# First attention half of a three-block kernel: state updates after even groups, outputs after odd ones, gate rows spread over more groups, products of queries and keys first

## The chip, the cores and the metric

The kernel runs on one core of one Trainium2 chip, in float32 (many matmul operands are split into two fp32r parts, "hi" and "lo", whose products are added). The metric is the device time of one execution in microseconds. The core has TensorE (PE) for matrix products, VectorE (DVE), ScalarE (ACT) and GpSimd (POOL) for element-wise work, and SyncE (SP), which here only issues DMA transfers. Each engine works through its own list of instructions in program order; they meet through semaphores that one engine increments and another waits for.

## The reference, cut to what matters

```
# attention: 2 batches, 8 heads, 768 tokens, head size 40
for t in range(S):
    m_new = maximum(f_gate[t] + m, i_gate[t])
    f_stab = exp(f_gate[t] + m - m_new); i_stab = exp(i_gate[t] - m_new)
    C = f_stab * C + i_stab * outer(v[t], k[t])
    n = f_stab * n + i_stab * k[t]
    h = C @ q[t];  denom = maximum(abs(n . q[t]), 1)
    y[t] = sigmoid(o_gate[t]) * h / denom
# first block: mixes tokens, then channels (x is y of all heads, 768 x 320 per batch)
h = relu(xT @ w_tok1) @ w_tok2;  u = x + hT
x = u + relu(u @ w_ch1) @ w_ch2
# second block: a 2-D Fourier transform, a layer norm, two channel layers
u = x + real(fft2(x));  un = (u - mean) / sqrt(var + 1e-6)
out = u + relu(un @ w_ch1') @ w_ch2'
```

## The kernel before

The recurrence over 768 tokens is worked out in chunks of 128 tokens: 6 chunks per batch, `cc` = 0 to 11 (`NCC`), the first six being batch 0. A chunk has two groups of 4 heads, so there are 24 groups `n` (`NG`); `cc = n // 2`, `g = n % 2`. The change lies in groups 0 to 11, batch 0 ("the first half").

For one group, in the order of the data:

- `log_weights(n)` on TensorE (lines 438 and 442): a mask and the product of two small matrices `L` and `R`, which hold the gates' logarithms, into one PSUM bank.
- `attend(n)` on ScalarE: the exponential of that bank is `W` (line 831). There is one such bank, so `log_weights(n + 1)` waits until `W` of group n is out of it.
- `products(n)` on TensorE (line 456): keys times queries, into one of two banks, so it waits until `scores(n - 2)` has read that bank.
- `scores(n)` on VectorE (line 1112): `S`, product times weight. `S` and `W` have two buffers each.
- `in_chunk(n)` on TensorE (line 480): `S` times the values, into the output bank of the chunk. `from_state(cc)` (line 465) adds what the state gives, `to_state(cc)` (line 489) makes the state's increment, `decays(cc)` (line 518) the decay factors.
- `update_state(cc)` on VectorE (lines 1103, 1105) adds the increment to `C`, after `to_state(cc)`. `finish(cc)` on VectorE (lines 1076 to 1087, five instructions) divides and gates the output: the finished rows of `xt`.
- `result_hi(cc)` on ScalarE (line 823) and `result_lo(cc)` on GpSimd (line 1390) split these rows into `x_hi` and `x_lo`, which `mix_tokens` on TensorE (line 533) reads.

The gates are prepared in three parts of 256 tokens by `gate_rows(part, step)` on VectorE, steps 0 to 8 (lines 1013 to 1046); part 2 is spread over groups by the table `GATE_AT`, which gives for a group n the steps that follow its scores. `spread_rows(cc)` (line 1062) makes `R` for a chunk, `spread(cc)` on ScalarE (line 797, for the second half also line 800) makes `L`. ScalarE and GpSimd also split the weights of the later layers piece by piece (lines 772 and 1397, table `SPLIT_AT`). At group 7 ScalarE has three more copies of 8 x 768 (lines 853 to 855).

TensorE begins with `WARM_UP` = 7 matmuls on constant data (line 627). Its loop over n of the first half is: `log_weights(n + 2)`, `products(n + 2)`, for odd n `from_state`, then `in_chunk(n)`, for even n `decays`, for odd n `to_state` and (from n = 5 on) `mix_tokens(0, (n - 5) / 2)`. From group 12 on, the order is written out between layers of the first block, and the PSUM bank of the log weights gets its mask by a copy on ScalarE (line 835) that `log_weights` waits for.

VectorE's loop over n of the first half is: `scores(n)`; `rest(n)`, which for even n is `update_state(cc - 1)` and `finish(cc - 1)` and for odd n nothing; the gate rows of `GATE_AT`; for odd n below 9 `spread_rows((n + 3) // 2)`.

SyncE issues the loads of a chunk in order: keys and queries, scaled queries, values and keys (`load_kv`, waits for `to_state` of two chunks before), the output gate `og` (line 348), then pieces of weights. `gate(cc)` on ScalarE (line 808) waits for `og`.

Of the kernel before, what the change touches and what calls it, by code (L numbers as in the profile page):

```python
# [19 lines left out]
NC = S // CH  # L20
# [21 lines left out]
LN_STEPS = 2 * 6 + 1  # L42
FOLD_STEPS = 18
NEG = -1.0e30
WARM_UP = 7
FCH = [F1 // P] * NBLK + [F2 // P] * NBLK
FBASE = [sum(FCH[:k]) for k in range(2 * NBLK)]
GATE_PARTS = [(0, 2 * CH), (2 * CH, 4 * CH), (4 * CH, S)]
PART_OF = [0, 0, 1, 1, 2, 2]

SP_PIECES = {2: (2,), 3: (3,), 4: (4, 5), 5: (6, 7, 8), 6: (9, 10), 7: (11, 12), 8: (13, 14)}
GATE_AT = {1: (0,), 2: (1, 2), 3: (3, 4), 4: (5, 6), 5: (7, 8)}
SPLIT_AT = {2: (0,), 3: (1,), 4: (2,), 5: (3,), 6: (4,), 7: (5,), 8: (6,), 9: (7,), 10: (8,), 11: (9,), 13: (10,),
            14: (11, 12, 13), 15: (14,), 16: (15,), 17: (16, 17), 18: (18,)}
SPLIT_L1 = {1: 14, 2: 15, 4: 16, 6: 17, 7: 18}
# [38 lines left out]
def build(nc, a, out):  # L94
# [220 lines left out]
    with block:  # L315
# [111 lines left out]
        def _(pe):  # L427
# [199 lines left out]
                pe.matmul(BANK[n], W[0][:, 0], W[0][:, :, :].rearrange("p a b -> p (a b)"),  # L627
                          start=True, stop=True).then_inc(warm_done, 1)
            pe.wait_ge(const_ready, 2)
            for n in range(2):  # L630
                log_weights(n)
                products(n)
            for n in range(NG // 2):
                c, g = n // 2, n % 2
                if 1 <= n <= NG // 2 - 2:
# [115 lines left out]
        def _(act):  # L751
# [73 lines left out]
            def attend(n):  # L825
                cc, g = n // 2, n % 2
                act.wait_ge(logw_done, n + 1)
                if n >= 2:
                    act.wait_ge(s_done, n - 1)
                    act.wait_ge(kw_done, kw_count(n - 2))  # L830
                act.activation(W[n % 2][:, :, :].rearrange("p a b -> p (a b)"), D_BANK,
                               ACT.Exp).then_inc(w_done, 1)
                if NG // 2 - 1 <= n < NG - 1:
                    act.wait_ge(w_done, n + 1)
                    act.activation(D_BANK.rearrange("p (a b) -> p a b", b=P),
                                   f32(mask[:, :]).unsqueeze(1).to_broadcast([P, 4, P]),
                                   ACT.Copy).then_inc(mask_done, 1)
                if g == 0 and 1 <= cc < NC:
                    decay(cc)
                if n == 0:  # L840
                    select()
                if n == 0:
                    gate(0)
                if n == 1:
                    gates_hi(1)
                if n == 2:
                    sources_hi(1)
                if n == 5:
                    gates_hi(2)
                if n == 6:  # L850
                    sources_hi(2)
                if n == 7:
                    act.activation(g_ah[32:32 + H, :], g_A[32:32 + H, :], ACT.Copy).then_inc(ah_done, 1)
                    act.activation(AB[1][0:H, :], g_A[32:32 + H, :], ACT.Copy).then_inc(ab_hi, 1)
                    act.activation(AB[1][64:64 + H, :], f32(g_bh[32:32 + H, :]), ACT.Copy).then_inc(ab_hi, 1)
                if n == 9:
                    act.activation(g_ea[32:32 + H, :], g_A[32:32 + H, :], ACT.Exp).then_inc(ea_ready, 1)
                if g == 0 and cc >= 1:
                    gate(cc)
                    if cc + 1 < NCC:  # L860
                        spread(cc + 1)
                if g == 0 and 2 <= cc <= NC:
                    result_hi(cc - 2)
                if g == 1 and cc >= NC:
                    result_hi(cc - 1)
                for m in SPLIT_AT.get(n, ()):
                    if m < N_CH2:
                        split_hi(m)
# [125 lines left out]
        def _(dve):  # L994
# [120 lines left out]
            def rest(n, parts=range(2)):  # L1115

                cc, c, g = n // 2, n // 2 % NC, n % 2
                for part in parts:
                    if g == 0 and part == 0 and c >= 1:
                        update_state(cc - 1)  # L1120
                    if g == 0 and part == 1 and cc >= 1:
                        finish(cc - 1)
# [49 lines left out]
            for n in range(NG // 2):  # L1172
                scores(n)
                if n == 0:
                    for step in range(4, 9):
                        gate_rows(1, step)
                rest(n)
                for step in GATE_AT.get(n, ()):
                    gate_rows(2, step)
                if n % 2 == 1 and n < 9:  # L1180
                    spread_rows((n + 3) // 2)
                if n == 7:
                    dve.wait_ge(ab_zero, 2)
                    dve.tensor_tensor(AB[1][96:96 + H, :], g_i[32:32 + H, :], f32(g_bh[32:32 + H, :]),
                                      ALU.subtract).then_inc(gate_step, 1)
                if n == 9:
                    dve.wait_ge(ah_done, len(GATE_PARTS) + 1)
                    dve.tensor_tensor(AB[1][32:32 + H, :], g_A[32:32 + H, :], f32(g_ah[32:32 + H, :]),
                                      ALU.subtract).then_inc(gate_step, 1)
# [168 lines left out]
        def _(pool):  # L1358
# [40 lines left out]
            def attend(n):  # L1399
                cc, c, g = n // 2, n // 2 % NC, n % 2  # L1400
# [14 lines left out]
                    scale_state(cc)  # L1415
                if g == 1 and cc >= NC and c < NC - 1:
                    scale_q(cc + 1)
                if g == 0 and 2 <= cc <= NC:
                    result_lo(cc - 2)
                if g == 1 and cc >= NC:  # L1420
                    result_lo(cc - 1)
# [83 lines left out]
```

## Time and profile before

| | us |
|---|---|
| runs of the kernel before | 402.97, 394.94, 400.56; median 400.56 |
| the profiled execution, its own time | 398.74 |
| its span, first to last instruction | 397.0 |
| TensorE busy in it | 387.6 (98%) |
| VectorE, ScalarE, GpSimd busy | 191.3, 151.6, 109.2 |
| mean granted TensorE clock | 0.986 |

A timeline row reads: start in us, duration in us, engine, line, operation, output <- input, sizes, xcount, and in brackets how long the engine sat idle before it and what ended the idle time. A float32 matmul appears as two records. A matmul's record reaches past the moment at which the next can start, because matmuls are pipelined. The granted clock is 1.00 for 2.4 GHz and 0.50 for 1.2 GHz.

### The profile page before, as it was taken

What the parts mean: (1) busy time and instruction counts of PE and PEld (TensorE: products, weight loads), DVE (VectorE), ACT (ScalarE), POOL (GpSimd) and SP (SyncE); (2) the same over time, 40 slices, a digit from 0 to 9 for tenths busy, and PEclk for the clock granted to TensorE, in tenths of its full rate; (3) what the DMA queues carried; (4) which work ended last, traced back from release to release, by engine and by line L of the source; (5) the groups of instructions that cost most, each with busy time, mean ns of one, the idle gap of its engine ahead of it and who ended that gap; (6) DMA issues with size and microseconds to landing.
All of it is one profiled execution on the core that took longest, in us unless ns stands there. A gap on an engine that the chain in (4) does not pass through costs nothing.

```text
span 397.0 us, 6364 instructions
## 1 busy us (share of the span) xinstructions
PE 387.6 (98%) x2482; PEld 371.2 (94%) x2482; DVE 191.3 (48%) x396; ACT 151.6 (38%) x312; POOL 109.2 (28%) x106
## 2 busy tenths in 40 slices
PE   8998989999999999999999999999999999999997
PEld 3888978999999999999999899999999989999996
DVE  7875655654443342147912555458924373340320
ACT  5656588577462131012631034505423201240310
POOL 5355596566332000000390000623550000000000
PEclk9995999999999999999999999999999999999999
DMA  6663688433130000032121000623130000000001
GB/s 170 194 184 119 209 293 259 163 97 106 35 101 17 18 0 0 18 117 99 23 95 35 0 2 0 217 78 120 10 142 0 2 1 35 17 2 35 17 7 44
DMA packets 18277, 30.54 MB, mean 77 GB/s; under 512 B 2504, under 2 KB 10824, under 8 KB 18248
## 3 DMA queue, kind: packets, MB, share of 16 engines
q1 hardware_dynamic: 17672, 29.87, 23.8%
q8 instruction: 20, 0.33, 0.4%
q10 hardware_dynamic: 576, 0.27, 0.2%
q14 instruction: 9, 0.07, 0.1%
HBM read 26.17 MB, written 3.96 MB: 76 GB/s over the span
## 4 chain that ended last, share of the span: by engine, by line
PE 93%; ACT 2%; issue 1%; POOL 1%; DVE 1%; DMA 1%; SPq 0%; ACTq 0%; DVEq 0%; POOLq 0%
PE ps L618 28%; PE ps L597 23%; PE ps L456 5%; PE ps L724 5%; PE ps L480 5%; PE ps L600 4%; PE ps L599 4%; PE ps L704 4%; PE ps L555 3%; PE ps L533 3%; PE ps L627 2%; PE ps L465 2%; PE ps L573 2%; PE ps L489 2%; PE ps L442 1%
## 5 line engine op out<-in xcount | busy, mean ns | idle before, releaser
L903 ACT ACTIVATE h_hi<-ps 128x384 fp32r<-128x384 f32 x88 | 43.3, 492 | 118.8 <-PE ps L600 118.8
L1153 DVE SCALAR_TENSOR_TENSOR h_lo<-ps,h_hi 128x384 fp32r<-128x384 f32 x88 | 48.7, 555 | 57.2 <-ACT h_hi L903 56.8
L1159 DVE TENSOR_TENSOR xt<-ps,xt 128x320 f32<-128x320 f32 x24 | 11.8, 491 | 72.0 <-PE ps L618 71.9
L618 PE MATMUL ps<-ch_hi,h_hi 128*128 128x320 f32 x144 | 45.5, 316 | 0.0
L618 PE MATMUL ps<-ch_hi,h_lo 128*128 128x320 f32 x144 | 44.5, 309 | 0.0
L618 PE MATMUL ps<-ch_lo,h_hi 128*128 128x320 f32 x144 | 44.5, 309 | 0.0
L618 PE MATMUL ps<-m_hi,h_hi 128*128 128x320 f32 x120 | 37.5, 313 | 0.6 <-POOL m_lo L1397 0.6
L618 PE MATMUL ps<-m_hi,h_lo 128*128 128x320 f32 x120 | 37.1, 309 | 0.0
L618 PE MATMUL ps<-m_lo,h_hi 128*128 128x320 f32 x120 | 37.1, 309 | 0.0
L1397 POOL TENSOR_TENSOR m_lo<-m_raw,m_hi 128x640 fp32r<-128x640 f32 x11 | 18.1, 1668 | 56.2 <-ACT m_hi L772 56.2
L597 PE MATMUL ps<-uT_hi,ch_hi 128*128 128x384 f32 x96 | 33.0, 344 | 0.0
L597 PE MATMUL ps<-uT_hi,ch_lo 128*128 128x384 f32 x96 | 32.1, 335 | 0.0
L597 PE MATMUL ps<-uT_lo,ch_hi 128*128 128x384 f32 x96 | 32.1, 334 | 0.0
L1112 DVE TENSOR_TENSOR S<-ps,W 128x512 f32<-128x512 f32 x24 | 16.5, 685 | 25.9 <-PE ps L456 17.4
L456 PE MATMUL ps<-qz,kT 128*128 128x256 f32 x96 | 27.5, 411 | 1.4 <-DVE S L1112 1.4
L480 PEld LDWEIGHTS ps<-vs,S 128*128 128x128 f32 x192 | 25.4, 199 | 2.0 <-issue 1.3
L618 PEld LDWEIGHTS ps<-ch_lo,h_hi 128*128 128x128 f32 x144 | 27.1, 188 | 0.1
L618 PEld LDWEIGHTS ps<-ch_hi,h_hi 128*128 128x128 f32 x144 | 27.1, 188 | 0.1
L618 PEld LDWEIGHTS ps<-ch_hi,h_lo 128*128 128x128 f32 x144 | 27.0, 188 | 0.0
L597 PE MATMUL ps<-uT_lo,m_hi 128*128 128x384 f32 x80 | 26.8, 335 | 0.0
L597 PE MATMUL ps<-uT_hi,m_lo 128*128 128x384 f32 x80 | 26.8, 335 | 0.0
L597 PE MATMUL ps<-uT_hi,m_hi 128*128 128x384 f32 x80 | 26.8, 335 | 0.0
(157 smaller groups left out, 924.0 us busy)
## 6 DMA issues: line engine op xcount, KB each, us to landing
ch_raw<-in_ch SPq DMA_DIRECT2D x11, 384.0 KB, 5.4
m_raw<-in_m SPq DMA_DIRECT2D x11, 320.0 KB, 4.5
vs<-in_vs SPq DMA_DIRECT2D x12, 168.0 KB, 2.7
kT<-in_kT SPq DMA_DIRECT2D x24, 80.0 KB
qz<-in_qT SPq DMA_DIRECT2D x24, 80.0 KB
ks<-in_ks SPq DMA_DIRECT2D x12, 160.0 KB, 3.3
og<-in_o SPq DMA_DIRECT2D x12, 160.0 KB, 3.4
x_scratch<-xt SPq DMA_DIRECT2D x12, 160.0 KB, 1.8
```

The costliest lines, as they stand in the source:

```text
L456: mm = pe.matmul(p_bank(n)[:, j * 2 * CH:(j + 1) * 2 * CH], kT[:, t, 2 * g + j], qz[:, t, :, 2 * g + j], start=True, stop=True)
L480: mm = pe.matmul(y_bank(cc)[:, head * DV:(head + 1) * DV], Sx[n % 2][:, j], vs[:, cc % 2, head], start=(head == 0), stop=True, skip_group_ ...
L597: pe.matmul(bank, w[wx][:, f, dc * P:(dc + 1) * P], ux[:, dc], start=(i == 0), stop=False)
L599: pe.matmul(bank, w[0][:, f, 2 * P:3 * P], uT_x[:, :], start=False, stop=False)
L600: pe.matmul(bank, w[1][:, f, 2 * P:3 * P], uT_x[:, :], start=False, stop=True).then_inc(l1_done, 1)
L618: mm = pe.matmul(bank, h[hx][:, f, i * P:(i + 1) * P], w[wx][:, f], start=(f == 0 and hx == 0 and wx == 0), stop=(f == FCH[k] - 1 and hx = ...
L704: mm = pe.matmul(bank[0:rows_, dst:dst + n], eo[yx][:, y, start:start + rows_], seq[wx][:, first:first + n], start=(i == 0), stop=(i == le ...
L724: mm = pe.matmul(R_BANK[n % 4][:, 0:DM], UT[ux][0:rows_, m, jp * P:(jp + 1) * P], chan[wx][0:rows_, m], start=(m == 0 and ux == 0 and wx = ...
L903: act.activation(h[0][:, f], h_bank(k, f), ACT.Relu).then_inc(hhi_done, 1)
L1112: dve.tensor_tensor(Sx[n % 2][:, :, :].rearrange("p a b -> p (a b)"), p_bank(n), W[n % 2][:, :, :].rearrange("p a b -> p (a b)"), ALU.mult ...
L1153: dve.scalar_tensor_tensor(out=h[1][:, f], in0=h_bank(k, f), scalar=0.0, in1=f32(h[0][:, f]), op0=ALU.max, op1=ALU.subtract).then_inc(hlo_ ...
L1397: pool.tensor_tensor(lo, raw, f32(hi), ALU.subtract).then_inc(wlo_done, 1)
```

## The change

Four edits in the first half. The warm-up has 5 matmuls instead of 7, and after it TensorE does the products of groups 0 and 1 and then both log weights, instead of alternating. VectorE does `update_state` after the scores of an even group and `finish` after those of the odd group that follows. The gate rows of part 2 and the `spread_rows` are distributed anew (`GATE_AT`, `SPREAD_AT`; `spread_rows(2)` moves from after group 1 to after group 0). The splits of finished rows (`result_hi`, `result_lo`) of chunks 0 to 3 move one group later on ScalarE and GpSimd.

```
--- before.py
+++ after.py
@@ -42,14 +42,15 @@
-WARM_UP = 7
+WARM_UP = 5
...
-GATE_AT = {1: (0,), 2: (1, 2), 3: (3, 4), 4: (5, 6), 5: (7, 8)}
+GATE_AT = {1: (0,), 2: (1, 2), 3: (3,), 4: (4, 5, 6), 5: (7, 8)}
+SPREAD_AT = {3: 3, 5: 4, 7: 5}
...
@@ -627,9 +628,10 @@
             pe.wait_ge(const_ready, 2)
-            for n in range(2):
-                log_weights(n)
-                products(n)
+            products(0)
+            products(1)
+            log_weights(0)
+            log_weights(1)
...
@@ -859,7 +861,7 @@
-                if g == 0 and 2 <= cc <= NC:
+                if (g == 1 and 2 <= cc < NC) or (g == 0 and cc == NC):
                     result_hi(cc - 2)
...
@@ -1174,11 +1176,15 @@
                 if n == 0:
                     for step in range(4, 9):
                         gate_rows(1, step)
-                rest(n)
+                    spread_rows(2)
+                if n % 2 == 0 and n > 0:
+                    update_state(n // 2 - 1)
                 for step in GATE_AT.get(n, ()):
                     gate_rows(2, step)
-                if n % 2 == 1 and n < 9:
-                    spread_rows((n + 3) // 2)
+                if n % 2 == 1 and n > 1:
+                    finish(n // 2 - 1)
+                if n in SPREAD_AT:
+                    spread_rows(SPREAD_AT[n])
...
@@ -1415,7 +1421,7 @@
-                if g == 0 and 2 <= cc <= NC:
+                if (g == 1 and 2 <= cc < NC) or (g == 0 and cc == NC):
                     result_lo(cc - 2)
```

First place, TensorE at the start of the program. Before (`W_94` is the constant tile of the warm-up, `S_96` the scores of group 0):

```order
L627 MATMUL ps<-W_94 128x512 x7
L438 MATMUL ps<-mask,identr 128x512
L442 MATMUL ps<-R,L 128x512
L456 MATMUL ps<-qz,kT 128x256 x2
L438 MATMUL ps<-mask,identr 128x512
L442 MATMUL ps<-R,L 128x512
L456 MATMUL ps<-qz,kT 128x256 x2
L480 MATMUL ps<-vs,S_96 128x42 x4
```

The same place in the changed kernel, where line numbers are higher by one:

```order
L628 MATMUL ps<-W_94 128x512 x5
L457 MATMUL ps<-qz,kT 128x256 x4
L439 MATMUL ps<-mask,identr 128x512
L443 MATMUL ps<-R,L 128x512
L439 MATMUL ps<-mask,identr 128x512
L443 MATMUL ps<-R,L 128x512
L481 MATMUL ps<-vs,S_96 128x42 x4
```

The two warm-up matmuls are gone, and nothing stands between the two log weights now.

Second place, VectorE from the state update after group 4 to the scores of group 5 (`S_97` is the scores' buffer of odd groups; the five rows to `xt` are `finish(1)`, the two to `g_bh` are gate steps 5 and 6). Before:

```order
L1105 TENSOR_TENSOR C<-ps,C 40x4x42 x2
L1076 TENSOR_SCALAR den<-ps 128x8
L1078 SCALAR_TENSOR_TENSOR den<-ps,den 128x8
L1081 RECIPROCAL rden<-den 128x8
L1083 TENSOR_TENSOR ps<-ps,rden 128x8x40
L1087 SCALAR_TENSOR_TENSOR xt<-xe_101,ps 128x320
L1034 TENSOR_TENSOR g_fi<-g_fi,g_A 40x256
L1037 CAST g_bh<-g_fi 40x256
L1112 TENSOR_TENSOR S_97<-ps,W_95 128x512
```

The changed kernel, from the same state update:

```order
L1107 TENSOR_TENSOR C<-ps,C 40x4x42 x2
L1033 TENSOR_TENSOR g_fi<-g_fi,g_m 40x256
L1036 TENSOR_TENSOR g_fi<-g_fi,g_A 40x256
L1039 CAST g_bh<-g_fi 40x256
L1114 TENSOR_TENSOR S_97<-ps,W_95 128x512
L1044 TENSOR_TENSOR AB_102<-g_fi,g_bh 8x256
L1048 TENSOR_TENSOR AB_102<-g_A,AB_102 8x256
L1078 TENSOR_SCALAR den<-ps 128x8
L1080 SCALAR_TENSOR_TENSOR den<-ps,den 128x8
```

Five rows moved from ahead of the scores to behind them, and one gate row (step 4) came in ahead.

Third place, GpSimd in groups 4 to 6 (`kw` are weighted keys, `C` the scaling of the state that waits for `from_state(2)`, `tok_lo` a piece of weights). Before:

```order
L1408 TENSOR_TENSOR kw_91<-ks,W_94 128x4x40
L1379 TENSOR_TENSOR qs<-qs,eAb 104x512
L1390 TENSOR_TENSOR x_lo<-xt,x_hi 128x320
L1397 TENSOR_TENSOR tok_lo<-tok_raw,tok_hi 128x384
L1408 TENSOR_TENSOR kw_91<-ks,W_95 128x4x40
L1385 TENSOR_TENSOR C<-C,eAb 104x336
L1397 TENSOR_TENSOR tok_lo<-tok_raw,tok_hi 128x384
L1408 TENSOR_TENSOR kw_92<-ks,W_94 128x4x40
```

The changed kernel:

```order
L1414 TENSOR_TENSOR kw_91<-ks,W_94 128x4x40
L1385 TENSOR_TENSOR qs<-qs,eAb 104x512
L1403 TENSOR_TENSOR tok_lo<-tok_raw,tok_hi 128x384
L1414 TENSOR_TENSOR kw_91<-ks,W_95 128x4x40
L1391 TENSOR_TENSOR C<-C,eAb 104x336
L1396 TENSOR_TENSOR x_lo<-xt,x_hi 128x320
L1403 TENSOR_TENSOR tok_lo<-tok_raw,tok_hi 128x384
L1414 TENSOR_TENSOR kw_92<-ks,W_94 128x4x40
```

The `x_lo` split now stands behind the scaling of the state, which itself waits for TensorE's `from_state` of group 5.

## Rows read from the trace of the kernel before

**Rows 1.** The page: its head and the granted clock in 40 slices

```profile
span 397.0 us, 6364 instructions
...
PEclk9995999999999999999999999999999999999999
```

**Rows 2.** Waits of TensorE over the whole run: us in total, times, longest

```profile
PE ps L442 <- ACT ps L835: 1.6, 1, 1.6
...
PE ps L456 <- DVE S L1112: 1.4, 1, 1.4
...
PE ps L438 <- ACT W L831: 0.5, 1, 0.5
```

**Rows 3.** Stages: length, busy time (count) by engine, granted clock, DMA share, GB/s

```profile
31.00:32.00 1.00, 0.99 (x2) 0.83 (x3) 0.94 (x3) 0.86 (x3) 0.00 (x0) 0.53 0.69 251
...
41.00:42.00 1.00, 1.00 (x10) 0.97 (x8) 0.97 (x2) 0.00 (x0) 0.00 (x0) 0.85 0.88 302
```

**Rows 4.** Timeline of VectorE: an early cast; state update of group 4 to scores 5

```profile
6.94 0.29 DVE L1037 CAST g_bh<-g_fi 40x256 fp32r<-40x256 f32 x1
...
26.46 0.69 DVE L1105 TENSOR_TENSOR C<-ps,C 40x168 f32<-40x168 f32 x2 [1.59 <-PE ps L489]
...
28.43 0.49 DVE L1087 SCALAR_TENSOR_TENSOR xt<-xe,ps 128x320 f32<-128x320 f32 x1
...
29.38 0.97 DVE L1037 CAST g_bh<-g_fi 40x256 fp32r<-40x256 f32 x1
30.28 0.67 DVE L1112 TENSOR_TENSOR S<-ps,W 128x512 f32<-128x512 f32 x1
```

**Rows 5.** Timeline of TensorE: products 7, log weights 9, products 9, mixing, log weights 11

```profile
31.01 2.07 PE L456 MATMUL ps<-qz,kT 128*128 128x256 f32 x4 [1.39 <-DVE S L1112]
...
42.53 0.40 PE L438 MATMUL ps<-mask,identr 128*128 128x512 f32 x1
...
42.99 1.02 PE L456 MATMUL ps<-qz,kT 128*128 128x256 f32 x4
...
46.30 0.39 PE L533 MATMUL ps<-x_hi,tok_hi 128*128 128x320 f32 x1
...
49.51 0.40 PE L438 MATMUL ps<-mask,identr 128*128 128x512 f32 x1
```

**Rows 6.** The start: chain piece of products 0; timeline of VectorE; products 3

```profile
11.01 0.86 PE ps L456 x4
...
12.15 0.66 DVE L1112 TENSOR_TENSOR S<-ps,W 128x512 f32<-128x512 f32 x1
...
15.12 0.69 DVE L1112 TENSOR_TENSOR S<-ps,W 128x512 f32<-128x512 f32 x1
...
16.39 0.66 DVE L1062 TENSOR_TENSOR R<-AB,roles 40x512 fp32r<-40x512 f32 x1
...
16.27 1.02 PE L456 MATMUL ps<-qz,kT 128*128 128x256 f32 x4
```

**Rows 7.** Timeline: GpSimd's state scaling of group 7, its x_lo 4; mixing that reads it

```profile
44.96 0.76 POOL L1385 TENSOR_TENSOR C<-C,eAb 104x336 f32<-104x336 f32 x1 [4.61 <-PE ps L465]
...
60.74 0.86 POOL L1390 TENSOR_TENSOR x_lo<-xt,x_hi 128x320 fp32r<-128x320 f32 x1 [1.06 <-ACT x_hi L823]
...
61.90 0.50 PE L533 MATMUL ps<-x_hi,tok_hi 128*128 128x320 f32 x1
```

**Rows 8.** Timeline of ScalarE in groups 6 and 7; below it pieces of the chain

```profile
30.83 0.47 ACT L808 ACTIVATE xe<-og 128x320 f32<-128x320 f32 x1
...
32.94 0.58 ACT L831 ACTIVATE W<-ps 128x512 f32<-128x512 f32 x1
33.54 0.84 ACT L853 ACTIVATE g_ah<-g_A 8x768 fp32r<-8x768 f32 x1
...
53.17 0.36 ACT x_hi L823
...
55.52 0.47 PE ps L442
```

## The prediction

> **What bounds the kernel now.** I read the page first: a span of 397.0 us, and a granted clock that is full in every slice but one [rows 1]. TensorE is busy 98% of the span, so only its idle time and its slow time can be won. The waits of TensorE come next: three matter in the first 60 us, 1.4 us of products for VectorE's scores, 0.5 us for ScalarE's weights `W`, 1.6 us for ScalarE's mask copy [rows 2]. The table of stages places the slow slice: the granted clock is 0.53 in the microsecond from 31 and back at 0.85 in the one from 41 [rows 3]. So for 10 us TensorE ran at 1.2 GHz, the lower of its two levels, after having been at 2.4 GHz. What it did just before is the 1.39 us wait of products 7, which began only at 31.01 [rows 5]. The wait and the slow stretch are one event: this is where the change acts.
>
> The cause of the wait is VectorE's queue. It got the state increment at 26.46, and had to do the update (to 27.15), `finish(1)` (to 28.92) and two gate rows before the scores of group 5, which ran from 30.28 to 30.95 [rows 4]. Products 7 needs these scores because it reuses their bank. TensorE had been free for it since 31.01 - 1.39 = 29.62.
>
> **The change, part by part.** All positions are in the time scale of the trace of before.
>
> *The start.* Two warm-up matmuls go. Each streams as many columns as one pair of products, 0.86 us in the chain [rows 6]; two products move into their place, so the first log weights come about when they did. TensorE now idles between log weights 0 and 1 for one exponential, and `in_chunk(0)` waits for scores 0, which VectorE cannot begin before 12.15: end 12.81, against a start of about 13.1 before. That gives 0.3 us. Against it, `spread_rows(2)` (0.66 us) now stands before scores 1, which then end at 15.81 + 0.66 = 16.5 instead of 15.8, and products 3, which started at 16.27, waits for them 0.2 us [rows 6]. What ends the 0.5 us wait for `W` a little later is ScalarE's chain behind the decays, which starts 0.3 us sooner. With the two splits gone from group 4 and `finish(0)` gone from ahead of scores 3 (a stall under 0.2 us), I take -0.4 us up to group 5; the bounds are 0 (ScalarE is held by the DMA of `og` anyway) and -0.9 (the whole 0.5 us of the wait and 0.4 besides).
>
> *The wait and the slow clock.* In group 4 VectorE now does update, gate steps 4, 5 and 6, then scores 5. `finish` took 28.92 - 27.15 = 1.77 us, and about 0.4 us for step 4 come in, so the scores end near 30.95 - 1.77 + 0.4 = 29.6, and sooner by what the cast loses less. The cast took 0.97 us here and 0.29 us in the first part of the gates [rows 4], so the scores end between 28.9 and 29.6: just before TensorE wants them at 29.62 (both move with the start). Sum: -1.4 us.
> Of that cast the Trainium skill says more (SBUF — State Buffer, Who interferes with whom): such a cast and a GpSimd instruction exclude each other for a whole instruction. By this rule the cast may again meet a GpSimd multiplication and cost the long time; then up to 0.2 us of wait stay; by the short one, none.
> If TensorE doesn't idle there, the clock should stay at 2.4 GHz. What that gives is read from equal work at both levels: from products 7 to log weights 9 it took 42.53 - 31.01 = 11.52 us, from products 9 to log weights 11 49.51 - 42.99 = 6.52 us [rows 5]. So -5.0 us. Bounds: 0, if the clock falls anyway, and -5.0.
>
> *`x_lo` becomes late.* `mix_tokens` in an odd group needs `x_lo` of that chunk. It used to be made a group earlier. Now GpSimd first waits for `from_state`, scales the state, then splits. In group 7 the scaling started at 44.96 and took 0.76; behind it 0.86 of `x_lo` [rows 7] ends at 46.6, while mixing started at 46.30 [rows 5]. So mixing waits 0.3 us in groups 5, 7 and 9. In group 5 this counts: +0.3. In 7 and 9 it lies inside the wait below. Bounds 0 and +0.9.
>
> *ScalarE in groups 6 to 8.* With the clock kept, TensorE is back for log weights 9 early: 29.2 + 6.52 + 0.3 = 36.0. They need `W` of group 8. ScalarE's `gate(3)` started at 30.83 and `W` of group 7 at 32.94, with a split of 0.36 between that is gone: 1.75 us. `gate(3)` hangs on `og`, whose load follows TensorE by 0.4 us less: 30.4. So `W` 7 runs 32.15 to 32.65; then three copies of 0.84 with their gaps (2.6), the moved split (0.36), a weight piece (0.4): `W` 8 from 36.0 to 36.5 [rows 8]. TensorE waits 0.5 to 0.6 us where it waited for nothing. +0.55; bounds 0 and +1.
>
> *The wait for the mask.* Log weights 12 started at 55.52. The chain to them runs from `to_state(3)` by way of the DMA of `og` and ScalarE's row of `x_hi` (0.36), `W` and mask [rows 8]. `to_state(3)` moves with all else, and the 0.36 leaves this chain: -0.36. The 1.6 us of wait shrink by more than that, because TensorE also arrives later by the two waits for `x_lo`; that is no further gain.
>
> *Given back behind it.* GpSimd used that 1.6 us. Now ScalarE's `x_hi` of chunk 4 and with it `x_lo`, which ended at 61.60 while mixing began at 61.90 [rows 7], come about 0.7 us later against TensorE: +0.4; bounds 0 and +1. Behind that, the loads and splits hang on TensorE's own progress and keep their distances.
>
> Sum: -0.4 - 1.4 - 5.0 + 0.3 + 0.55 - 0.36 + 0.4 = -5.9 us. The profiled execution took 398.74 (its span and 1.7 around it), so 392.8. Against the median of 400.56 that is 1.9% less; the profiled execution lies 1.8 below that median. The spread of the runs, 394.94 to 402.97, fits a clock that falls for a different time in each: without the fall the profiled one would be 393.7.
>
> **The rivals.**
>
> *The clock falls anyway, in the same place or near it.* For it: the margin of scores 5 is 0 to 0.7 us, and other waits remain (0.5, 0.5, 0.4). Against it: the waits of 1.6 and 0.5 us in this trace left the clock full. Time: only the small terms remain, -0.4 - 1.4 + 0.3 - 0.36 = -1.9, so 396.9; with the wait still there 398.3.
>
> *A short fall at the start.* Warm-up and products end sooner, and TensorE then idles for about 0.7 us (the exponential of group 0) and 0.5 us (scores 0) within two microseconds. A fall as short as half of that seen would cost 2.5 us of TensorE time and some of the slack there: about 395.
> The Trainium skill has a rule that speaks for it (TensorE: Matmul & The Clock Gate, What's actually happening): the low clock is the default, and activity releases it; two warm-up matmuls less are less activity. The trace shows the clock going down at 31, behind idle time.
>
> *Slower than before.* The same idle time at the start, but the clock doesn't come back until mixing begins. What speaks for it: after 31.01 products, `from_state`, `in_chunk` and `to_state` at 1.2 GHz did not bring it back; it came back after the first mixing, log weights and products had run in a row [rows 3, 5]. Before group 5 there is no mixing at all. A fall at 14 that lasts through group 5 would double 18 us of TensorE work: +10 or more after the slack, about 403. It decides from some 16 us of slow clock on.
>
> *The whole is hidden.* If ScalarE, not TensorE, paced groups 5 to 9, the freed clock would turn into waits: the 0.55 would be 3 or more. Its list in two groups is about 5 us of 7, so this is unlikely; 396.
>
> **How the numbers follow.** The sum as worked out: 0.62, own range 390.5 to 395 (its bounds together: -8.2 to -3.7). Clock falls anyway: 0.14. Short fall at the start: 0.12. Hidden by ScalarE: 0.06. Slower: 0.06. The forecast is 392.8. The range of 390.3 to 398 leaves out the slow case and a little of the two ends. Two per cent is about what a measurement of this kernel can tell; it lies at 392.5, inside the likeliest case. Half of that case, and a bit, is faster by over 2%: 0.36; within 2%: 0.57; slower by over 2%: 0.07.
>
> **What would show it.** Right: no slice with a clock below full behind the warm-up; no wait of products 7 for scores; waits of about 0.3 us of mixing for `x_lo` in groups 5, 7, 9 and one of about 0.5 us of log weights for `W` near 36; the wait for the mask copy under 1 us; log weights 12 near 49.4 instead of 55.5. Wrong: a clock of 0.5 anywhere from 10 to 60 us; products 0 that wait for their DMA; a wait for `W` or `x_lo` over 1 us.

## The result, and the profile after

| | before | after |
|---|---|---|
| runs side by side, us | 402.97, 394.94, 400.56, 401.70; median 401.13 | 405.52, 404.42, 405.77, 405.23; median 405.38 |
| the profiled execution: time, span, mean granted clock | 398.74, 397.0, 0.986 | 405.52, 403.7, 0.979 |

The ratio is 1.0211 (95% interval 1.0136 to 1.0286): slower by 1.4 to 2.9%, where 392.8 had been forecast. In the experiments below the kernel before ran 68 times more. It has two kinds of time: 28 runs, with a mean granted clock of 0.996 to 1.0 (no fall, or one of some 3 us), took 394.0 to 397.2 us, and 40 runs, with a clock of 0.966 to 0.987, took 399.0 to 408.0. The profiled execution of before is one of the second kind. (The ratios given below leave out runs of either kernel that lie more than 1.5% above its fastest; where falls of the clock matter, all times are given.)

The head of the page of the changed kernel and its clock in 40 slices of 10.1 us, to be held against [rows 1]:

```profile
span 403.7 us, 6357 instructions
...
PEclk9999965999999999999999999999999999999999
```

The slow slice in the fourth place is gone, as forecast. There is another one instead, longer, from 50 us on. Two stages of the changed kernel (length; busy time and count of PE, PEld, DVE, ACT, POOL; granted clock; DMA share; GB/s) bound it:

```profile
53.90:71.20 17.30, 15.69 (x62) 14.78 (x63) 3.83 (x9) 7.58 (x17) 10.03 (x10) 0.51 0.63 205
71.00:71.50 0.50, 0.50 (x7) 0.50 (x7) 0.00 (x0) 0.50 (x2) 0.34 (x1) 1.00 0.56 156
```

So TensorE ran at 1.2 GHz for 17.3 us, where before it did for 10. At the full clock the same work takes half: 8.65 us, if nothing else limits. 405.5 - 8.65 = 396.9 would be left, and the changed kernel takes 396.2 to 396.8 when its clock is kept up (experiments below). Waits of TensorE in the changed kernel (us in total, times, longest), against [rows 2]:

```profile
PE ps L457 <- DMA qz<-in_qT: 1.9, 2, 1.7
PE ps L439 <- ACT W L833: 1.8, 4, 0.7
...
PE ps L443 <- ACT ps L837: 1.1, 1, 1.1
PE ps L439 <- DVE R L1064: 0.8, 1, 0.8
PE ps L457 <- DVE S L1114: 0.8, 1, 0.8
PE ps L534 <- POOL x_lo L1396: 0.5, 3, 0.2
```

The first line is a wait of 1.7 us for a load of queries; the matmuls of the kernel before never waited for one. Timeline of TensorE in the changed kernel, against [rows 5] and the log weights 12 of [rows 8]: products 7, log weights 8, log weights 9, log weights 12, products 12, and the first mixing of the token layer's way back:

```profile
31.04 1.13 PE L457 MATMUL ps<-qz,kT 128*128 128x256 f32 x4 [0.77 <-DVE S L1114]
...
36.30 0.47 PE L439 MATMUL ps<-mask,identr 128*128 128x512 f32 x1 [0.80 <-DVE R L1064]
...
39.99 0.50 PE L439 MATMUL ps<-mask,identr 128*128 128x512 f32 x1 [0.58 <-ACT W L833]
...
53.34 0.47 PE L443 MATMUL ps<-R,L 128*128 128x512 f32 x1 [1.06 <-ACT ps L837]
55.51 2.08 PE L457 MATMUL ps<-qz,kT 128*128 128x256 f32 x4 [1.69 <-DMA qz<-in_qT]
...
77.96 0.50 PE L556 MATMUL ps<-hp_hi,tok_hi 128*128 128x320 f32 x1
```

Log weights 12 come 2.2 us earlier than before (55.52), although TensorE had 5.0 us to win. Then two waits stand in a row, 1.06 and 1.69 us with half a microsecond of work between. The second runs from 53.82 to 55.51. Stages of 0.2 us (the clock is the third number from the end) say when the clock fell:

```profile
53.60:53.80 0.20, 0.20 (x1) 0.00 (x0) 0.20 (x1) 0.20 (x1) 0.20 (x2) 1.00 1.01 334
53.80:54.00 0.20, 0.02 (x1) 0.00 (x0) 0.17 (x1) 0.20 (x1) 0.20 (x1) 0.58 0.92 269
```

It fell as the second wait began. So in this execution the wait of 1.69 us didn't bring it down; ahead of the fall stand the 1.06 us and 0.18 us for `x_lo`. The second wait only lies in the slow stretch. At the last line the kernel is 6.8 us behind (before: 71.18), and the span ends 6.7 us later. The chain of waits says what the wait for the load is (start, us, what):

```profile
48.75 0.33 SPq L332
49.08 0.04 issue
49.12 6.35 DMA qz<-in_qT
55.47 0.04 issue
55.51 1.65 PE ps L457 x3
```

SyncE issued the load at 49.12, behind three loads of `ch_raw` of 384 KB each (45.50 to 47.92), and it took 6.35 us to land. In the kernel before the same load was issued at 51.06, and products 12 started at 56.00. It landed with nothing to spare: the tile view of `qz` in the kernel before lists, as idle time before its users,

```profile
  DMA qz<-in_qT: 0.3, 1
```

a wait of a weight load of 0.3 us. That cover of zero was overlooked. Now VectorE, GpSimd and ScalarE of the changed kernel around 31, against [rows 4] and [rows 8]:

```profile
27.31 1.34 DVE L1033 TENSOR_TENSOR g_fi<-g_fi,g_m 40x256 f32<-40x256 f32 x1
28.68 1.10 DVE L1036 TENSOR_TENSOR g_fi<-g_fi,g_A 40x256 f32<-40x256 f32 x1
29.82 0.44 DVE L1039 CAST g_bh<-g_fi 40x256 fp32r<-40x256 f32 x1
30.29 0.69 DVE L1114 TENSOR_TENSOR S<-ps,W 128x512 f32<-128x512 f32 x1
...
33.56 2.64 DVE L1064 TENSOR_TENSOR R<-AB,roles 40x512 fp32r<-40x512 f32 x1
...
33.11 0.75 POOL L1391 TENSOR_TENSOR C<-C,eAb 104x336 f32<-104x336 f32 x1 [2.99 <-PE ps L466]
33.82 0.86 POOL L1396 TENSOR_TENSOR x_lo<-xt,x_hi 128x320 fp32r<-128x320 f32 x1
34.64 1.01 POOL L1403 TENSOR_TENSOR tok_lo<-tok_raw,tok_hi 128x384 fp32r<-128x384 f32 x1
...
33.73 0.47 ACT L810 ACTIVATE xe<-og 128x320 f32<-128x320 f32 x1 [2.86 <-DVE xt L1089]
```

Three things stand in these rows. Scores 5 start at 30.29, as before (30.28), though `finish(1)` is out of their way: the two gate steps ahead of them took 1.34 and 1.10 us, three times what the same steps of an earlier part take in this trace (0.39 and 0.42 at 6.30 and 6.72), beside GpSimd instructions from 27.09 to 30.11. The `R` row of chunk 4 took 2.64 us instead of 0.68. And `gate(3)` on ScalarE waited 2.86 us for `finish(1)`, which now comes after scores 5; before it started at 30.83.

### The profile page after: what moved, and what is told of

The parts are those of the page before. It is cut to its first block, busy times and chain, and to the rows that moved or that the text cites. A ratio compares the mean times of both kernels' runs of the same rounds, so it can differ in the third digit from the quotient of the medians.

```text
span 403.7 us, 6357 instructions
## 1 busy us (share of the span) xinstructions
PE 389.8 (97%) x2478; PEld 372.7 (92%) x2478; DVE 194.8 (48%) x396; ACT 151.3 (37%) x312; POOL 109.8 (27%) x106
## 4 chain that ended last, share of the span: by engine, by line
PE 86%; ACT 2%; DVE 2%; DMA 2%; issue 2%; POOL 1%; SPq 1%; ACTq 0%; DVEq 0%; POOLq 0%
PE ps L619 28%; PE ps L598 23%; PE ps L726 5%; PE ps L481 4%; PE ps L457 4%; PE ps L601 4%; PE ps L600 4%; PE ps L706 4%; PE ps L534 3%; PE ps L556 3%; PE ps L466 2%; PE ps L574 2%; DMA qz<-in_qT 2%; PE ps L490 1%; POOL m_lo L1403 1%
## 5 line engine op out<-in xcount | busy, mean ns | idle before, releaser
L481 PEld LDWEIGHTS ps<-vs,S 128*128 128x128 f32 x192 | 27.4, 213 | 3.6 <-issue 2.8
L481 PE MATMUL ps<-vs,S 128*128 128x42 f32 x192 | 27.0, 296 | 1.9 <-DVE S L1114 1.1
```

The lines of the kernel that those rows point to most:

```text
L481: mm = pe.matmul(y_bank(cc)[:, head * DV:(head + 1) * DV], Sx[n % 2][:, j], vs[:, cc % 2, head], start=(head == 0), stop=True, skip_group_ ...
```

## The experiments

All kernels compute the whole result. "The kernel with a cure" below has two additions. The keys and queries of chunk 6 are issued ahead of the weight pieces. And TensorE fills idle places with spare matmuls of 512 columns into a PSUM bank that is overwritten later, some before products 7 and some before log weights 12. Times are us, with the mean granted clock in brackets where it matters.

### The change, one part at a time

The start alone (in the kernel before):

```
-WARM_UP = 7
+WARM_UP = 5
-            for n in range(2):
-                log_weights(n)
-                products(n)
+            products(0)
+            products(1)
+            log_weights(0)
+            log_weights(1)
```

> The kernel before with only the start changed (5 warm-up matmuls, both products first). Theory A (the loss of the changed kernel is the 17 us at 1.2 GHz behind the wait of products 12 for the load of keys and queries, and this wait comes from TensorE arriving there earlier by its vector order): the start matters little, the fall at 31 us stays, 399 to 402 us, ratio 0.99 to 1.01. Rival B (the thinner start is what sets the clock on another course for the rest): the clock falls at 54 us here too and the time is near 405, ratio 1.01 to 1.02.

Measured: 394.25, 394.63 (1.0), 401.16, 401.68 (0.983): two runs of each kind, as before. The profiled one is of the first kind. Its waits of TensorE:

```profile
PE ps L442 <- ACT ps L836: 1.4, 1, 1.4
PE ps L456 <- DVE S L1113: 1.4, 1, 1.4
```

and the clock of its page:

```profile
PEclk9999999999999999999999999999999999999999
```

Products 7 waited the same 1.39 us as in [rows 5], log weights 12 waited 1.41 us, and the clock stayed full. So behind a wait of this size the clock falls in some executions and not in others. (The two runs of 401 have no profile; where their clock fell isn't known.) The start alone is no cause of 405.

VectorE's new order with its gate tables alone:

```
-GATE_AT = {1: (0,), 2: (1, 2), 3: (3, 4), 4: (5, 6), 5: (7, 8)}
+GATE_AT = {1: (0,), 2: (1, 2), 3: (3,), 4: (4, 5, 6), 5: (7, 8)}
+SPREAD_AT = {3: 3, 5: 4, 7: 5}
...
-                rest(n)
+                if n % 2 == 0 and n > 0:
+                    update_state(n // 2 - 1)
...
+                if n % 2 == 1 and n > 1:
+                    finish(n // 2 - 1)
+                if n in SPREAD_AT:
+                    spread_rows(SPREAD_AT[n])
```

> The kernel before with only VectorE's list changed (state updates behind even groups, outputs behind odd ones, gate rows and spreads as in the changed kernel); start and splits as before. Theory A: no fall at 31 us, products 12 waits over 1 us for keys and queries, the clock falls near 54 us, 403 to 406 us, ratio 1.005 to 1.02. Rival B: with the old start no fall at 54 us, 393 to 396 us, ratio 0.98.

Measured: 403.65 to 404.74 in all four runs (0.979 to 0.983), ratio 1.0224 (1.0189 to 1.0258). This part alone makes the loss. Log weights 12 waited 1.72 us for the mask at 53.40 and products 12 another 0.69 for the load at 54.56; the clock fell at 55.2, after products 12 had begun, and was back at 68.8.

The later splits alone:

```
-                if g == 0 and 2 <= cc <= NC:
+                if (g == 1 and 2 <= cc < NC) or (g == 0 and cc == NC):
```

> The kernel before with only the splits of finished rows one group later on ScalarE and GpSimd. Both theories: the fall at 31 us stays; mixing waits up to 0.3 us for x_lo in groups 5, 7, 9, the mask chain to log weights 12 is 0.36 us shorter; 399 to 402 us, ratio 0.995 to 1.005.

Measured, ten runs: four at 394.06 to 394.55 (1.0), six at 399.58 to 403.13; median 399.65, ratio 1.0018 (0.9944 to 1.0092). No effect. Mixing waited three times for `x_lo`, 0.5 us together. Its profiled run (403.13) shows the late load at products 12 in a kernel with VectorE's old order. Timeline of SyncE and TensorE of it:

```profile
46.22 0.33 SPq L332 DMA_DIRECT2D qz<-in_qT  x1
...
50.29 0.47 PE L442 MATMUL ps<-R,L 128*128 128x512 f32 x1 [0.39 <-ACT ps L835]
53.38 2.08 PE L456 MATMUL ps<-qz,kT 128*128 128x256 f32 x4 [2.62 <-DMA qz<-in_qT]
```

Here no clock fell at 31, TensorE came early, and the load took over 7 us from its issue. The clock fell inside this wait, at 51.3, half a microsecond after it began at 50.76. In the run of the start alone the same load, issued at 46.41, let products 12 start at 51.40, 4.99 us later. There too it landed just in time (a weight load waited 0.15 us for it). What makes the difference of two microseconds is open.

### The load at products 12

The changed kernel with the keys and queries of chunk 6 ahead of the weight pieces:

```
             for cc in range(2, NCC):
-                load_qk(cc)
+                if cc != NC:
+                    load_qk(cc)
...
                 load_o(cc)
+                if cc == NC - 1:
+                    load_qk(NC)
                 for n in SP_PIECES
```

> The changed kernel, but SyncE issues the keys and queries of chunk 6 ahead of the three weight loads of chunk 5 instead of behind them. Theory A: products 12 no longer waits, only the 1.06 us for the mask copy is left, the clock stays full from there: 17.1 us at half speed and 1.7 us of wait go, 395 to 398 us, ratio 0.985 to 0.995. Rival C (the wait for the mask copy, or ScalarE's own late loads, make the clock fall with or without this wait): 403 to 406 us.

Measured, ten runs: 396.30, 396.49, 396.77, 397.93 (0.996 to 1.0), 399.46, 400.11 (0.991), 402.89 to 404.22 in four (0.979 to 0.983); median 399.78, ratio 1.0060 (1.0022 to 1.0098). The wait for the load is gone, and now the clock stays up in some runs. In the profiled one (404.22) log weights 12 waited 1.64 us for the mask, and it still fell, at 55.35, after products 12 had begun without a wait. Two stages of it, the start and the stretch behind that wait:

```profile
10.00:20.00 10.00, 8.93 (x45) 7.27 (x44) 7.32 (x15) 5.69 (x13) 3.11 (x4) 0.83 0.65 191
56.00:69.00 13.00, 13.00 (x53) 12.37 (x52) 3.32 (x8) 5.95 (x14) 8.55 (x9) 0.50 0.65 219
```

So the fall doesn't need the wait for the load: four of ten runs are as slow as the profiled one, in which the mask wait alone stands before the fall, and two more fell for a shorter time (where is not known). With the load late as well, all eight runs of the changed kernel and of VectorE's order alone took 403.6 or more. These counts suggest that the load makes the long fall likelier; they are too few to show it. The first row is a short fall at the start, of which more below.

The opposite, the kernel before with these loads behind the next `load_kv`, which makes them late:

```
                 load_kv(cc)
+                if cc == NC:
+                    load_qk(cc)
                 load_o(cc)
```

> The kernel before, with only the keys and queries of chunk 6 issued later, behind the values and keys of that chunk: products 12 must wait 2 to 3 us for them. Theory A (this wait behind the mask wait is what makes the clock fall in every run): every run falls near 54 us, 402 to 407 us, no run under 399; ratio 1.005 to 1.02. Rival H (the wait only costs its own length): half of the runs stay near 396 to 397, the others near 403.

Measured: 403.71, 404.70, 405.08, 408.03 (0.966 to 0.979), ratio 1.0194 (1.0122 to 1.0266). Timeline of TensorE:

```profile
52.49 0.47 PE L445 MATMUL ps<-R,L 128*128 128x512 f32 x1 [1.07 <-ACT ps L838]
56.51 2.08 PE L459 MATMUL ps<-qz,kT 128*128 128x256 f32 x4 [3.55 <-DMA qz<-in_qT]
```

The clock fell at 55.15, inside the second wait (52.96 to 56.51), and was 0.58 on average from 57 to 71, after a short fall at 31 had already cost this profile some time (0.83 from 30 to 40). With the old order and the old start, a mask wait of 1.07 and a load wait behind it are enough: no run is of the first kind, and all four take 403.7 or more, as only 2 of the 19 runs of the kernel before beside them do. The load wait is longer here than in the changed kernel, and here the clock fell inside it, there ahead of it. So this shows that such waits can do it, not the size of each share.

### The idle places filled

The kernel before with the cure (six spare matmuls at each place):

```
+            def keep_busy(bank, count):
+                for _ in range(count):
+                    pe.matmul(bank, identr[:, :], mask[:, :].unsqueeze(1).to_broadcast([P, 4, P]),
+                              start=True, stop=True, skip_group_check=True)
...
+                    if n == 10:
+                        pe.wait_ge(s_done, 11)
+                        keep_busy(BANK[0], 6)
                     log_weights(n + 2)
+                    if n == 5:
+                        keep_busy(BANK[6], 6)
                     products(n + 2)
```

> The kernel before, with TensorE kept busy where it waited: 6 spare matmuls of 512 columns (1.3 us at full clock) ahead of products 7 and 6 ahead of log weights 12, and the keys and queries of chunk 6 issued ahead of the weight loads. Theory D (the clock falls because of idle time at these two places, by chance in some runs, because the same wait falls differently each time): no run with a fall, every run 393.5 to 396 us, clock 1.000; ratio to before about 0.985. Rival E (the sparse small matmuls around the waits, not the idle time, make it fall): about half of the runs still fall and take 399 to 404 us.

Measured, ten runs: 394.46 to 396.74, median 395.16, clock 0.996 to 1.0 in all. The kernel before ran 19 times beside it, 394.77 to 405.20, median 399.32; the ratio is 0.9942 (0.9900 to 0.9985), where 5 of the 12 runs of before that count had a fall. Timeline of TensorE at the two places:

```profile
29.62 1.55 PE L638 MATMUL ps<-mask,identr 128*128 128x512 f32 x6
...
49.90 1.55 PE L638 MATMUL ps<-mask,identr 128*128 128x512 f32 x6
```

Work of 1.55 us stands where TensorE waited 1.4 and 1.6 us, and it costs nothing: the seven runs of the kernel before without a long fall, 394.77 to 397.18 (median 395.38), are no faster. No run has a long fall (a clock of 0.996, in one, leaves room for some 3 us of 1.2 GHz). The cure also moves a load, which alone could be what helps at the second place. The changed kernel separates the two: with the load moved alone, four of ten runs took 402.9 or more, and with the spare matmuls as well (next run) none of ten took over 399.4. So it is the idle time of TensorE that brings the clock down.

The changed kernel with the cure (three spare matmuls before products 7, six before log weights 12; the diff is the same otherwise):

> The changed kernel with the same cure: 3 spare matmuls ahead of products 7 (its wait is 0.77 us), 6 ahead of log weights 12, keys and queries of chunk 6 first. Theory D: no fall in any run, every run 395.5 to 397.5 us, that is 1 to 3 us slower than the kernel before with the cure: this difference is what the new order itself costs on VectorE, ScalarE and GpSimd. Rival E: falls in half of the runs, 399 to 404 us. If the order itself costs nothing, it is within 0.5 us of the kernel before with the cure.

Measured, ten runs: 396.21 to 399.42, median 397.78 (0.991 to 1.0), ratio 0.9992 (0.9949 to 1.0036). The 405 is gone, but the kernel isn't level with the one above: 396.2 at best against 394.5. Two more short falls are in its profile. Two stages of it:

```profile
13.70:17.20 3.50, 3.50 (x12) 2.95 (x12) 3.28 (x8) 0.60 (x1) 0.46 (x1) 0.52 0.59 211
37.50:41.00 3.50, 3.45 (x11) 2.89 (x11) 3.23 (x10) 3.43 (x6) 2.89 (x4) 0.51 0.91 285
```

The first stands behind 0.69 us idle before log weights 1 and 0.76 before `in_chunk(0)`; the second behind the 0.79 that log weights 8 waited for the slow `R` row. (In the profile of the changed kernel itself the waits at these three places were 0.69, 1.08 and 0.80 us, and the clock stayed full.)

The same with the old start:

> The changed kernel with the cure, but the start of before: 7 warm-up matmuls, log weights and products alternating. Theory M (the clock of 0.50 from 13.7 to 17.2 us in the cured changed kernel comes from the two idle stretches of the thinner start): no run falls there, all runs 395.8 to 397.5 us, clock at least 0.995; the median drops by 1 to 2 us from 397.8. Rival N (the remaining falls all come from the wait for the R rows near 37 us): the median stays at 397 to 398.

Measured, nine runs: 396.12 to 398.79, median 396.88; clock 0.999 to 1.0 in eight of them, 0.996 in one; ratio 1.0043 (1.0022 to 1.0064). The start's short fall goes with the new start. Log weights 8 still waited 0.79 us for the `R` row in the profile, without a fall. At the full clock the new order still costs 1.5 to 2 us: 1.7 against the 395.16 of the kernel before with the cure, measured in another session, 2.0 against the runs without a fall beside it (median 394.9).

### What the new order costs at the full clock

A third buffer for `xe`, so that `gate(3)` doesn't wait for `finish(1)`:

```
-    xe = [at(f"xe{t}", o + 44736 + 1280 * t, [P, DM]) for t in range(2)]
+    xe = [at(f"xe{t}", (o + 44736, o + 46016, R_U + 3072)[t], [P, DM]) for t in range(3)]
...
-                if cc >= 2:
-                    act.wait_ge(x_done, cc - 1)
+                if cc >= 3:
+                    act.wait_ge(x_done, cc - 2 if cc < NC else cc - 1)
```

> The changed kernel with the cure and a third buffer for the gated outputs of the first half, so that gate(3) on ScalarE no longer waits for finish(1) on VectorE. Theory F (the order's own cost is the wait of gate(3), 2.9 us on ScalarE, which makes W of groups 7 and 8 late): the waits of TensorE for W at log weights 6 and 9 shrink under 0.3 us each, 0.5 to 1 us faster than the changed kernel with the cure alone. Rival G (the cost lies in VectorE's gate and R rows, which take 2 us more beside GpSimd): no difference, within 0.3 us.

Measured: 401.50 to 402.81 (0.983 to 0.987), median 402.59, ratio 1.0118 (1.0059 to 1.0177): worse. Timeline of ScalarE, VectorE and TensorE, where times are 1.7 us later than in the changed kernel:

```profile
32.44 0.47 ACT L823 ACTIVATE xe<-og 128x320 f32<-128x320 f32 x1
...
35.26 4.28 DVE L1077 TENSOR_TENSOR R<-AB,roles 40x512 fp32r<-40x512 f32 x1
...
39.63 0.47 PE L442 MATMUL ps<-mask,identr 128*128 128x512 f32 x1 [2.43 <-issue]
```

ScalarE is early, as wanted. But the `R` row, which began at 35.26, now got its turn behind five GpSimd instructions (34.81 to 38.99) and not behind three, and ended only at 39.54. The profile names nobody for the 2.43 us that log weights 8 waited; they started 0.09 us after the row's end, and they read it. The clock fell at 41.2. Why the row came behind five and not three is not shown; the fourth, `kw`, took 0.46 us here and 0.91 in the changed kernel with the cure, where `W` of its group came late.

The `R` rows ahead of `finish`, where GpSimd is idle (it waits for `from_state`):

```
+                if n in SPREAD_AT:
+                    spread_rows(SPREAD_AT[n])
                 if n % 2 == 1 and n > 1:
                     finish(n // 2 - 1)
-                if n in SPREAD_AT:
-                    spread_rows(SPREAD_AT[n])
```

> The changed kernel with the cure (spare matmuls, keys and queries first), and VectorE makes the R rows before finish instead of behind it. Theory K (the R rows of group 5 took 2.64 us instead of 0.68 only because GpSimd ran three multiplications and subtractions beside them, and this makes log weights 8 wait 0.8 us): the R rows are done before GpSimd begins, 0.7 us long, the wait at log weights 8 is gone, and with it the short fall behind it; fast runs 395.3 to 396, about 0.8 us under the cured changed kernel's 396.2. Rival L (the rows are long whatever runs beside them, by their own data): 2.6 us again, 396 to 397.

Measured, nine runs: 396.46 to 400.99, median 397.99, ratio 1.0063 (1.0010 to 1.0116). Timeline of VectorE, ScalarE and TensorE:

```profile
31.88 0.68 DVE L1077 TENSOR_TENSOR R<-AB,roles 40x512 fp32r<-40x512 f32 x1
...
34.30 0.47 ACT L823 ACTIVATE xe<-og 128x320 f32<-128x320 f32 x1 [3.13 <-DVE xt L1102]
...
36.66 0.70 PE L442 MATMUL ps<-mask,identr 128*128 128x512 f32 x1 [1.19 <-ACT W L846]
```

The `R` row takes 0.68 us again and nobody waits for it. But `finish(1)` is later by it, so `gate(3)` and the weights `W` behind it are, and TensorE waits 1.19 us for these. The clock was at 1.2 GHz behind that wait, from 36.7 to 40.1.

The same with the old start and the old splits:

> Only VectorE's new order, R rows before finish, with the start and the splits of before and the cure. If VectorE's new order is worth anything once it does not collide with GpSimd: 394 to 395 us in all runs, 0.3 to 1 us under the kernel before with the cure (395.2 median). If finishing behind the odd groups costs on its own (gate(3) waits for finish(1)): 395.5 to 396.5.

Measured, nine runs: 397.35 to 400.85, median 398.17, ratio 1.0096 (1.0067 to 1.0124). `gate(3)` started at 34.62 and the log weights at 37.34 (group 8) waited 1.92 us for `W`; the clock fell at 38.3. The guess that this was the best form of the order was wrong.

Both together, with the old start and the splits of the changed kernel, and the cure:

> VectorE's new order, the new gate tables and the later splits, with the old start, and with all cures at once: keys and queries of chunk 6 loaded ahead, spare matmuls in the idle places, the R rows ahead of finish, and a third buffer for xe so that gate(3) doesn't wait for finish(1). Each of the last two was tried alone and left the time at 396 to 398 or more. Theory A, the new order's own cost is these two causes side by side, and removing one leaves the other: both gone, log weights 8 and 9 wait under 0.3 us each, and the runs lie at 394.3 to 395.5, level with the kernel of before that has spare matmuls (median 395.2). Theory B, a third cause (gate rows 1 us longer ahead of scores 5, or something not seen): 396 to 398 again, with a wait of TensorE that neither change touches.

Measured: 395.17, 394.71, 394.21, 394.34, clock 0.999 to 1.0 in all; the kernel before took 400.43 to 407.11 (median 401.91) in seven runs beside it; ratio 0.9792 (0.9718 to 0.9866), which compares with runs that all had a fall. Timeline of ScalarE, VectorE and TensorE:

```profile
30.87 0.47 ACT L822 ACTIVATE xe<-og 128x320 f32<-128x320 f32 x1
...
31.69 0.68 DVE L1076 TENSOR_TENSOR R<-AB,roles 40x512 fp32r<-40x512 f32 x1
...
35.85 1.77 DVE L1076 TENSOR_TENSOR R<-AB,roles 40x512 fp32r<-40x512 f32 x1
...
35.12 0.39 PE L442 MATMUL ps<-mask,identr 128*128 128x512 f32 x1
...
37.82 0.39 PE L442 MATMUL ps<-mask,identr 128*128 128x512 f32 x1
```

`gate(3)` is back where it was before (30.83), the `R` row is short, and neither log weights 8 nor 9 wait. (The next `R` row still takes 1.77 us, where nobody waits for it.) So these two causes were the own cost of the order, to within what runs of different sessions can tell. This kernel and the kernel before with the cure are the best two, both ahead of the kernel before and of the changed one. They were not run side by side. Both lie where the kernel before lies in its runs without a fall, 394.0 to 397.2: with the clock kept up, the new order gains nothing that these runs show.

## Why the prediction was wrong

**The bound of the kernel.** Right in the event (a wait of 1.39 us, then 10 us of slow clock), wrong in its reading as a fixed cost. This is the first step that failed. The prediction noted that the spread of the runs fits a clock that falls for a different time in each, and then counted -5.0 us in full, from one profiled execution of the slower kind. 28 of 68 runs of the kernel before have no fall, or one of 3 us, so there was next to nothing to win in them.

**The start, -0.4.** In the changed kernel `in_chunk(0)` started at 13.43 (forecast: 12.8; before: 13.12) behind a wait of 1.08 us for scores 0, which came 0.5 us late, and log weights 5 at 22.58, where they had started at 22.20: 0.4 us lost up to there, and not won. With the start alone they came at 22.07, so most of the forecast gain was not there even without the new order of VectorE. The rival of a short fall at the start was real: 3.5 us of slow clock in the profile of the changed kernel with the cure. In the profile of the changed kernel itself it didn't come, so it is no part of the 405.

**The wait, -1.4.** This step failed by its size. 1.77 us of `finish` were taken away, and step 4 was put in at 0.4. It took 1.34, and step 5 behind it, not counted as slower, 1.10 where it had taken 0.51. Scores 5 came when they had come before. The cast cost 0.44 us, not the long 0.97: the prediction looked for the stretching there, and it came in the two steps ahead. So a queue was shortened by one instruction, and the next ones took its time, since GpSimd was then at work beside them. TensorE started products 7 at 31.04 instead of the forecast 29.2, as late as before (31.01). Its wait is 0.77 us instead of 1.39 only because it had itself arrived 0.65 us later than before, after a wait for `W` of 0.32 at 26.86 and the loss at the start.

**The slow clock, -5.0.** Here it held: the clock stayed full at 31. The step that failed is behind it: the sum takes it that TensorE, once past products 7, keeps its clock, and has no term for a fall at the wait that it leaves standing. Log weights 12 were forecast at 49.4 and came at 53.34. They waited 1.06 us for the mask (forecast: "under 1 us"), and then the clock fell for 17.3 us, +8.65. The load at products 12 has no term either: "the loads and splits hang on TensorE's own progress and keep their distances". It had no slack, and took as long as its queue took, 4.9 to 7.1 us in these profiles: +1.69, inside the slow stretch. That the mask wait suffices for the long fall, and that it goes when TensorE is kept busy there, is shown by the runs; what the wait for the load adds is not. The 10 us fall was exchanged for a longer one, and one whose mean clock (0.979) is the same in all four runs.

**`x_lo`, +0.3.** The three waits came where forecast, 0.18 us each. **`W` in group 8, +0.55.** 0.58 measured, the right size, but at 39.99 and with another cause ahead of it: `gate(3)` waited for `finish(1)`, which the prediction had overlooked; it gave that wait to `og` alone. **The wait for the mask, -0.36, and what is given back behind it, +0.4**, can't be told apart in the slow stretch. **The `R` row of chunk 4** was not priced: 0.80 us of wait at log weights 8. The bounds of the single terms add up to -7.7 and not to the -8.2 at which the range of the sum begins; the other end, -3.7, fits.

**The rivals.** "The clock falls anyway" (0.14) was the right mechanism. It was priced at 396.9 because it counted only the loss of the same 5 us, not a fall in another place, from which the clock took 17 us to come back instead of 10. "Slower than before" had the right sign at 0.06, for a fall at 14 and not at 54. The argument against, "the waits of 1.6 and 0.5 us in this trace left the clock full", was one draw: in the profile of the changed kernel with the early load a wait of 1.64 at the same place was followed by the fall.

What stays open: what decides, for one and the same wait, whether the clock falls (behind 1.06 us it did, behind 1.55 in the profile of before it didn't); and why the load of queries takes 5 us in two profiles and 6.4 or 7.1 in others, behind the same three weight loads.

## What to carry to other kernels

Where the time of a kernel has two humps, the profile shows one of them: find out which, before a slow stretch in it is counted as a gain. A few spare matmuls in the place of an idle stretch of a microsecond cost nothing here, show whether the clock is the cause, and were the cure. And set the fall against the waits to a fraction of a microsecond before one of them is called its cause: here the longer wait, and the more striking one, began as the clock fell. When work is pulled forward, list every load and every two-input VectorE instruction that it is pulled towards, and ask of each how much slack it had.

## What the runs showed of the hardware

A wait of TensorE of 1.39 us at the full clock was followed by 1.2 GHz in the profile of the kernel before and not in that of the start alone; 1.64 us was followed by it (changed kernel, load early), 1.55 (before) and 1.41 (start alone) were not. With two waits close together, 1.06 and 1.69, 1.72 and 0.69, 1.07 and 3.55 us in the profiled run, it came in every run of these three kernels, 12 of 12. In the first of these the clock fell as the second wait began, in the second after it, and in the third inside it. The Trainium skill (TensorE: Matmul & The Clock Gate, What's actually happening) says of the start of a kernel that the point at which the clock is released differs from run to run of one kernel. No run here shows that for the start; the falls in the middle differ likewise: the kernel before took 394.0 to 397.2 us in 28 of 68 runs, and 399.0 to 408.0 in the others.

VectorE instructions with both inputs in SBUF stretch beside GpSimd, and by several GpSimd instructions in a row, not only by one: the same `R` row took 0.68 us alone, 1.77 beside one GpSimd instruction, 2.64 beside three and 4.28 beside five, each time ending about 0.55 us after the last of them (the times of GpSimd are rough). The GpSimd instruction that followed was the longer one then, 1.46 us instead of 1.00 for the same split. Scores, which read one input from PSUM, took 0.65 to 0.69 us throughout. The Trainium skill (SBUF — State Buffer, Who interferes with whom) has the rule that an instruction with two SBUF inputs contends with a GpSimd instruction that reads SBUF; the trace agrees. What it adds is that VectorE doesn't always get its turn between two GpSimd instructions that follow without a gap.
